# Last expert tile of a mixture-of-experts kernel: high parts on ScalarE, down products per half and per column half; the last waits on SyncE, the scatter's limit in a register

## The reference

```python
logits = x @ w_gate
expert_idx = np.argmax(logits, axis=1)
...
for e in range(E):                       # E = 8
    mask = expert_idx == e
    xe = x[mask]
    h = np.maximum(xe @ w1[e], 0.0)      # 512 -> 1024
    ye = h @ w2[e]                       # 1024 -> 512
    out[mask] = gate_w[mask, None] * ye
```

## Time and profile before

| | |
|---|---|
| median of 3 runs | 819.56 us (818.15 to 820.72) |
| the profiled execution's own time | 819.36 us |
| its span, first to last instruction | 817.6 us |
| share of TensorE in the chain that ended last | 88% |
| busy: PE, DVE, ACT, POOL | 779.0, 564.1, 491.3, 455.6 us |
| granted TensorE clock, mean | 0.979 of full |
| granted TensorE clock, 800 to 810 us | 1.00 |

### The profile page before, as it was taken

The page is one execution under the profiler, slowest core; times in us unless marked ns, Lnnn a source line. Parts: engine busy times, 40 slices in busy tenths (PEclk is TensorE's granted clock), DMA queues, the critical chain, the costliest instruction groups (busy, mean ns, idle before and its releaser), DMA issues.

```text
span 817.6 us, 13322 instructions
## 1 busy us (share of the span) xinstructions
PE 779.0 (95%) x4255; PEld 688.7 (84%) x4255; DVE 564.1 (69%) x967; ACT 491.3 (60%) x973; POOL 455.6 (56%) x404
## 2 busy tenths in 40 slices
PE   6999999999998999999999999994999999999994
PEld 5899899899996889999999999893788888888883
DVE  4788888888896787877788777974454454454451
ACT  4678878878897998778778877944222224223000
POOL 3235265265157688458557644426885659765700
PEclk8899999999999999999999999995999999999998
DMA  9898988985840940950790050074672536460200
GB/s 197 177 209 170 204 173 169 209 168 130 201 148 23 309 160 2 352 176 1 245 375 27 1 206 1 14 259 159 202 239 61 205 133 216 142 234 24 85 14 19
DMA packets 71844, 123.43 MB, mean 151 GB/s; under 512 B 33343, under 2 KB 36127, under 8 KB 67681
## 3 DMA queue, kind: packets, MB, share of 16 engines
q1 hardware_dynamic: 64176, 90.71, 41.3%
q10 hardware_dynamic: 5056, 25.56, 9.4%
q0 software_dynamic: 2544, 6.31, 2.0%
HBM read 60.26 MB, written 34.24 MB: 116 GB/s over the span
## 4 chain that ended last, share of the span: by engine, by line
PE 88%; ACT 5%; DVE 3%; issue 2%; DMA 1%; POOL 1%; SPq 0%; ACTq 0%; POOLq 0%; DVEq 0%
PE ps L1390 7%; PE ps L1478 5%; PE ps L1480 5%; PE ps L1479 5%; PE ps L1512 5%; PE ps L1513 5%; PE ps L1511 5%; PE ps L1656 4%; PE ps L1657 4%; PE ps L1658 4%; PE ps L1682 4%; PE ps L1680 4%; PE ps L1681 4%; PE ps L1378 4%; PE ps L1379 4%; PE ps L1402 4%
## 5 line engine op out<-in xcount | busy, mean ns | idle before, releaser
L786 POOL TENSOR_TENSOR split<-wraw,split 128x512 f32 (+1 forms) x112 | 140.3, 1286 | 54.9 <-ACT split L947 51.4
L947 ACT ACTIVATE split<-wraw 128x512 f32 (+1 forms) x128 | 68.8, 618 | 142.0 <-PE ps L1658 65.9
L1111 DVE TENSOR_TENSOR ptl<-ps,pth 128x512 fp32r<-128x512 f32 x144 | 98.7, 686 | 36.1 <-ACT pth L881 34.1
L761 POOL TENSOR_TENSOR hw<-hw,ha 128x384 f32<-128x384 f32 x64 | 65.4, 1021 | 72.7 <-ACT hw L959 72.7
L881 ACT ACTIVATE pth<-ps 128x512 fp32r<-128x512 f32 x144 | 86.7, 602 | 31.4 <-PE ps L1390 31.3
L1091 DVE TENSOR_REDUCE negmax<-ps 128x1 f32<-128x768 f32 x96 | 91.0, 948 | 8.4 <-PE ps L1379 8.4
L872 ACT ACTIVATE pr<-ps,negmax 128x768 f32<-128x768 f32 x96 | 86.8, 904 | 6.8 <-DVE negmax L1091 6.8
L1390 PE MATMUL ps<-cst,pr 128*128 128x128 f32 x576 | 88.5, 274 | 1.1 <-ACT pr L872 1.1
L1478 PE MATMUL ps<-xh,wih 128*128 128x384 f32 x256 | 86.2, 337 | 1.0 <-DVE hp L1147 1.0
L1480 PE MATMUL ps<-xh,wil 128*128 128x384 f32 x256 | 86.3, 337 | 0.0
L1479 PE MATMUL ps<-xl,wih 128*128 128x384 f32 x256 | 85.9, 336 | 0.0
(11 more groups left out here) (205 smaller groups left out, 2008.9 us busy)
## 6 DMA issues: line engine op xcount, KB each, us to landing
routed<-blank SPq DMA_DIRECT2D x33, 771.0 KB, 13.6
wraw<-in_moe_w ACTq DMA_DIRECT2D x24, 1024.0 KB, 5.4
wraw<-in_moe_w SPq DMA_DIRECT2D x8, 1024.0 KB, 5.4
operand<-qk_hi SPq DMA_DIRECT2D x31, 192.0 KB, 4.2
operand<-qk_hi SPq DMA_DIRECT2D x15, 384.0 KB, 4.7
operand<-qk_lo SPq DMA_DIRECT2D x30, 192.0 KB, 4.3
operand<-mask SPq DMA_DIRECT2D x14, 384.0 KB, 5.0
xg<-routed SPq DMA_DIRECT2D x19, 256.0 KB
```

What stands on the lines that cost most here:

```text
L786: pool.tensor_tensor(split_piece(E_LO[x], ring, k), wraw[:, x, i, :], split_piece(E_HI[x], ring, k).bitcast(F32), ALU.subtract).then_inc(e ...
L1111: dve.tensor_tensor(ptl[:, at:at + CW], ps[:, 4 + c % 2, :], pth[:, at:at + CW].bitcast(F32), ALU.subtract).then_inc(ptl_done, 1)
```

## The change

Four things are changed, and all but one touch only tile 18.

1. The high part `hth` of tile 18 is made by ScalarE, one copy per half, in place of VectorE. VectorE makes only the low part.
2. `mm2(18)` is written out anew as `last_mm2`. The 512 output columns are cut into two halves of 256, in banks 2 and 0, so that there are 48 matmuls of 256 columns in place of 24 of 512. They start when the first half of `hth` is there: 16 matmuls with it, then 8 with the first half of `htl`, and then, after the wait for the second half, 12 for each column half. `y_out(18)` becomes two multiplications of 256 columns, one for each.
3. The twelve waits on `s_out` move from the end of GpSimd's program to the end of SyncE's.
4. `bounds_check` gets a register that is set once, in place of a number; with a number, each of the 19 scatters sets a register first (a MOVE).

```diff
@@ SyncE
             sp.wait_ge(s_xg[1], 32 * (NSLOT_TILES // 2))
+            for i in range(NYO):
+                sp.wait_ge(s_out[i], 16 * ((NSLOT_TILES - 1 - i) // NYO + 1))
@@ GpSimd
+            limit = pool.to_reg(NTOK - 1)
+
             def scatter(t):
-                pool.wait_ge(yo_done, t + 1)
+                pool.wait_ge(yo_done, t + (2 if t == NSLOT_TILES - 1 else 1))
                 pool.indirect_dma_start(out=out, ...
-                                        in_=yo[t % NYO][:, :], in_offset=None, bounds_check=NTOK - 1, oob_is_err=False).then_inc(s_out[t % NYO], 16)
+                                        in_=yo[t % NYO][:, :], in_offset=None, bounds_check=limit, oob_is_err=False).then_inc(s_out[t % NYO], 16)
...
-            for i in range(NYO):
-                pool.wait_ge(s_out[i], 16 * ((NSLOT_TILES - 1 - i) // NYO + 1))
@@ ScalarE
+            last = NSLOT_TILES - 1
+            for c in range(2):
+                act.wait_ge(ht_ready, 2 * last + c + 1)
+                act.activation(hth[:, 4 * c:4 * c + 4, :], ps[:, 4 + c, :].rearrange("p (k n) -> p k n", n=P), ACT.Copy).then_inc(ht_hi, 1)
@@ VectorE, h_in
-                    dve.tensor_copy(hth[:, ks, :], turned).then_inc(ht_hi, 1)
+                    if t < NSLOT_TILES - 1:
+                        dve.tensor_copy(hth[:, ks, :], turned).then_inc(ht_hi, 1)
@@ VectorE, end
-            y_out(NSLOT_TILES - 1)
+            t = NSLOT_TILES - 1
+            dve.wait_ge(s_out[t % NYO], 16 * (t // NYO))
+            for half, bank in enumerate(LAST_BANKS):
+                cols = slice(half * DM // 2, (half + 1) * DM // 2)
+                dve.wait_ge(mm2_done, t + half + 1)
+                dve.tensor_scalar(yo[t % NYO][:, cols], ps[:, bank, 0:DM // 2], gi[:, t, 0:1], None, ALU.mult).then_inc(yo_done, 1)
@@ TensorE, end
-            mm2(NSLOT_TILES - 1)
+            t = NSLOT_TILES - 1
+            wait(pe, yo_done, t - 1)
+            pe.wait_ge(e_lo[1], needs[t])
+
+            def last_mm2(kts, half, x):
+                cols = slice(half * DM // 2, (half + 1) * DM // 2)
+                bank = ps[:, LAST_BANKS[half], 0:DM // 2]
+                for kt in kts:
+                    if x == 0:
+                        pe.matmul(bank, hth[:, kt, :], weights(S_W2H, t, kt)[:, cols], start=(kt == 0), stop=False)
+                        pe.matmul(bank, hth[:, kt, :], weights(S_W2L, t, kt)[:, cols], start=False, stop=False)
+                    else:
+                        mm = pe.matmul(bank, htl[:, kt, :], weights(S_W2H, t, kt)[:, cols], start=False, stop=(kt == KF - 1))
+                        if kt == KF - 1:
+                            mm.then_inc(mm2_done, 1)
+
+            early, late = range(0, KF // 2), range(KF // 2, KF)
+            pe.wait_ge(ht_hi, 2 * t + 1)
+            last_mm2(early, 0, 0)
+            last_mm2(early, 1, 0)
+            pe.wait_ge(ht_done, 2 * t + 1)
+            last_mm2(early, 0, 1)
+            last_mm2(early, 1, 1)
+            pe.wait_ge(ht_done, 2 * t + 2)
+            for half in range(2):
+                last_mm2(late, half, 0)
+                last_mm2(late, half, 1)
```

More of the change, by code:

```diff
@@ L476, in build @@
         FIRST_SEL = (7, 6, 4, 5)
+        LAST_BANKS = (2, 0)
         def op_landed(p, o):
```

## The result

The changed kernel takes 813.72 us (median of 4 runs, 812.37 to 814.14) against 819.94 (4 runs, 818.15 to 820.72). The ratio is 0.9927, 95% interval 0.9914 to 0.9940: 6.2 us less, with bounds of 4.9 and 7.1. The profiled execution took 812.37 us, its span is 810.5.

The account below looks back on a forecast made before the run. Bound: the unoverlapped chain of waits in the last 18 us, then GpSimd's DRAIN. TensorE 1.99, VectorE 0.29, register 0.50 and moved waits 2.35 sum to 5.13 us off 819.36, giving 814.2, by median 814.4; range 812.6 to 817.7.

Parts of the forecast that it names:

- What bounds the kernel: Last 18 us: engines wait in turn without overlap, then GpSimd's waits and its 2.77 us DRAIN end the program.
- Start of the last product: TensorE starts tile 18's down product after ScalarE's copy of one half, at 801.62 instead of 804.00, 2.38 us earlier.
- 48 matmuls of 256 columns: Last down product: 0.122 us per matmul, 5.86 us in all; it ends 1.99 us earlier, cutting costs 0.4.
- the prediction's upper bound: Last product: sequencer limit of 0.141 us per matmul with a register instruction; 32 such matmuls add 0.6 us.
- `y_out` in halves: Last y_out: first half hidden behind TensorE, second takes 0.46 us instead of 0.75, saving 0.29 us.
- The register: Last scatter: without the MOVE it starts 0.28 us after the value it waits for, saving 0.50 us.
- the rival that the check of bounds costs the time: Last scatter: the delay belongs to the bounds check, so only 0.03 us go; register failing, chance 0.35.
- The waits: Program end: moving GpSimd's last waits to SyncE saves 2.35 us, with bounds of 0 and 2.35.
- The likeliest case: Program end: GpSimd's DRAIN is work of its own, 2.77 us from the scatter's end; 814.4 us, chance 0.50.
- Both rivals: DRAIN starts at the landing (816.1 us, chance 0.25), or ends 5.11 us behind the scatter regardless (816.8 us, chance 0.17).
- the rival that the prediction hung on it: Program end: DRAIN ends a fixed 5.11 us behind the scatter, so moving waits gains nothing; 816.8 us, chance 0.17.
- The narrow matmuls at a lower rate: Last product: 256 columns at a quarter rate give 830 us, at half rate 819.6; slow case, chance 0.05.

Follow-up runs that it names:

- the limit alone: Kernel before with only the scatter's bounds limit put in a register: 819.42 us against 819.5, ratio 0.9997 (0.9986 to 1.0007).
- The experiment with VectorE's copies: Changed kernel with tile 18's high parts made by VectorE again instead of ScalarE: 814.79 us against 818.62 before, ratio 0.9947.

## Why the prediction was right, step by step

**What bounds the kernel.** Right: the parts taken alone and together changed the tail by what they freed in the chain, but for the limit alone, where 0.3 of its 0.5 us were lost again at the meeting of the engines.

**Start of the last product.** Forecast 1.38 us behind the start of the transposes, measured 1.49. ScalarE's copy took 0.60 us as worked out; TensorE took 0.25 instead of 0.14 us behind it. The experiment with VectorE's copies shows that ScalarE gives 0.36 us, near the 0.32 named.

**48 matmuls of 256 columns.** Sum forecast 6.12 with the first one's delay, measured 6.34 (799.20 to 805.54). From the 25th on they took 0.120 us each (802.48 to 803.92 for twelve), the line through 384 and 512 columns being right. The first 16 took 2.32 us (799.20 to 801.52), 0.145 each on average. But that isn't a steady pace: 13 of the 16 steps are 0.12 or 0.13 us, and three are longer, the first two (0.28 and 0.22) and one in the middle (0.20). So the prediction's upper bound, 0.141 for each matmul with a register instruction, came out as a sum and not as the mechanism, which it gave to every such step. What makes the three steps long stays open. A sequencer that starts with no lead would fit the first two, and with 512 columns only the first step is longer (0.33 us, then 0.23); no run takes the register instructions away. TensorE's gain was 1.66 instead of 1.99 us.

The Trainium skill's figures for a stream ("TensorE: Matmul & The Clock Gate", section "Back-to-back issue gap") didn't hold here: by interpolation, an estimate, they give 98 ns for 256 columns, and 120 were measured.

**`y_out` in halves.** 0.48 instead of 0.46 us, the first hidden. But cut and halves together lose 0.27 us, as their two terms in the prediction (0.4 against 0.29) already hinted.

**The register.** 0.28 us, as taken; the rival that the check of bounds costs the time is out.

**The waits.** The likeliest case was right in its place and nearly in size: the DRAIN, not SyncE, ends the span, 3.02 us behind the scatter instead of 2.77. Both rivals are out in size: from the landing it would have been 4.4 us, at a fixed distance 5.1. But its description was incomplete. "Work of its own" is not a fixed price but 82 ns for each transfer, and an early DRAIN takes it off the path. Nor is it all that a DRAIN does: with one transfer to clear and this one on its way, it still ended only 1.7 us behind the scatter, so the landing, which the prediction left out of the DRAIN's time, can matter.

The Trainium skill's rule ("VectorE: DVE Perf Modes", section "The DRAIN you can't avoid") gives about 12 ns, constant on all engines, for the DRAINs at a program's start and end. That fits SyncE's 7 ns and not GpSimd's 135 to 2766 ns, and the rival that the prediction hung on it did not occur.

**The sum.** 5.13 us forecast for the tail, 4.57 measured. Short of the forecast are 0.11 at the start, 0.22 in the product, 0.02 in `y_out` and 0.25 in the DRAIN, less 0.03 won at the meeting of the engines. The median went the other way, by 6.2 us. The prediction has nothing for that: it took the one profiled execution of before as typical and the clock in the last product as 1.00, and in two of five traces with the 2.70 us gap it was not. That the forecast time of 814.4 us is met within 0.7 is therefore luck in part: a tail that gained 0.56 us less than forecast and a median that gained 1 to 2 us more than the tail cancel. The narrow matmuls at a lower rate, the rival on the other side, did not occur.

## What to carry to other kernels

When a pipeline runs dry at the end of a program, look past the last computation: here 5.3 of the last 17.4 us lay behind the last scatter's record, and GpSimd's DRAIN, with 33 transfers since the one before, was the largest item in them (2.77 us). In the three kernels with a DRAIN ahead of the last scatter, where GpSimd idles, it was over before the scatter was due, and it took up to 2.6 us off the end. To shorten TensorE's last gap, fill it with the tile before rather than cut matmuls in two: here the cut won 0.27 us at the seam and paid 0.6 in its matmuls.

## What the runs showed of the hardware

- GpSimd's DRAIN, when it starts behind all landings: 2766, 1617 and 135 ns with 33, 19 and 1 of its transfers since the last one, 82 ns each. When it starts with the last scatter still on its way, it ends 3.0 us behind the scatter's record with 33 to clear and 1.7 us with one; with 32 it ended 3.1 us behind in two executions and 4.2 in a third, and with 14, behind the scatters into the table, 3.0.
- After an idle gap of 2.70 us, in which the clock stood at 1.00 (2.4 GHz), TensorE's granted clock fell to 0.50 (1.2 GHz) during the next product in two of five executions, 0.9 us after the matmuls had gone on, and the product took 7.4 us instead of 5.73; after gaps under 1 us it fell in none of nine. That the gap is the cause is not shown.
- Matmuls of fp32r with 256, 384 and 512 columns run at 0.120, 0.176 and 0.228 to 0.231 us each. In the first 16 of 256 columns, with a register instruction ahead of each, 13 steps took 0.12 or 0.13 us and three 0.20 to 0.28.
- With the wait on a register's MOVE ahead of it, an indirect transfer started 0.78 us behind what it waited for; with the wait on the transfer itself 0.28 us.
